# A fused attention and two-MLP kernel: stacked hi/lo heads in the feature projection, folds moved from VectorE to GpSimd, weight work reordered

## The chip, the cores and the metric

The kernel runs on one core of a Trainium2 chip. The metric is the device time of one execution in microseconds (us), from which the median of several executions is quoted.

## What is computed

Three layers follow each other, for 4 batches of 576 tokens with 512 features.

```python
proj = einsum('bhsd,df->bhsf', x, w_phi)            # 8 heads of 64, 128 features
proj = proj - max(abs(proj), axis=-1)
phi  = concatenate([exp(proj), exp(-proj)])         # for q and for k
kv, z = phi(k)^T v, sum(phi(k))
attn = phi(q) kv / (phi(q) z + 1e-6)
x  = attn as (4, 576, 512)
u  = x + real(fft(fft(x, axis=1), axis=2))
x  = u + relu(layernorm(u) @ w_ch1) @ w_ch2         # 512 -> 2048 -> 512
u  = x + (relu(x^T @ w_tok1) @ w_tok2)^T            # over tokens, 576 -> 256 -> 576
out = u + relu(u @ w_ch1') @ w_ch2'                 # 512 -> 1536 -> 512
```

Nearly every product is made of three passes in the type fp32r: a number is split into a rounded part `hi` and a rest `lo`, and hi·hi, hi·lo and lo·hi are summed in PSUM.

## The kernel before, in words

**Attention** (`front`). Two heads of a batch make a pair; there are 16 pairs, four for a batch, and a step for each. All engines run the same list of steps, each in its own order, tied by semaphores. Step k on TensorE (`pe_step`, L421) projects the five token groups of pair k+1 (units REST, KA, KB, QA, QB; REST has one tile of 128 tokens, the others two, so nine tiles in a pair) and, between them, turns the query features of pair k (`pe_turn`), forms `kv` (`pe_kv`) and forms `num` (`pe_num`). The last two are in plain f32, for which one matmul of the program shows as two records in the trace. Between the units stand pieces of the Fourier transform of the batch before (`pe_piece`, in the steps where k % 4 is 1, 2 or 3).

In `pe_project` (L286) the 128 rows of a tile hold the features of both heads, and `wphi` is block diagonal, so 256 columns come out, 128 for each head. Three matmuls of 256 columns are made for a tile: hi with `wphi_hi`, hi with `wphi_lo`, lo with `wphi_hi`. `qk_hi` is rounded on ScalarE three steps ahead (`act_round`), `qk_lo` is the rest, made on GpSimd (`pool_split`). Each unit goes to one of two PSUM banks, so it waits (`shifted`) until VectorE has read the unit before the last one.

VectorE subtracts the largest absolute value (`dve_shift`), divides (`dve_norm`) and, for the transform, forms sums of mirrored tokens (`dve_sum`) and of mirrored features (`dve_even`); GpSimd forms the differences (`pool_fold`) and adds the finished transform to x (`pool_add`, `pool_row`). SyncE's queue issues the loads (`load_qk`, `load_v`) and the stores of u (`store`), in the order in which they are written, each behind its waits.

**First MLP** (`channel_mlp`, NF1 = 16 chunks j of hidden features; 6 blocks of 384 tokens). `early_vector` makes the mean and variance of block 0 (`early_stats`) and its reciprocal root and normed values (`early_norm`, which calls `dve_first_rstd`) while attention still runs. During block 0 the last batch's transform is still under way, and the weights come in: SyncE loads a chunk to one of four buffers, ScalarE rounds it (`act_weights`), GpSimd makes the rest (`mlp1["gpsimd"](pool, waits, first, stop)`). The sequence on GpSimd after the last step is written out in `gpsimd`:

```python
mlp1["gpsimd"](pool, (), 4, 6)
pool_add(pool, LAST, 0)
pool_add(pool, LAST, 1)
mlp1["gpsimd"](pool, ((7, u_stored[2], 32),), 6, 8)
pool_add(pool, LAST, 2)
pool_row(pool, LAST)
mlp1["gpsimd"](pool, ((13, u_stored[3], 32),), 8)
```

**Token MLP** (`token_mlp`). Its second weight `w2` is loaded by SyncE once all of the first MLP's outputs are made (`y_done`), into memory that the first MLP's weights held, then rounded on ScalarE and split on VectorE; TensorE's second product waits for it.

## Time and profile before

| | us |
|---|---|
| median of 3 runs (lowest, highest) | 994.19 (993.21, 994.72) |
| the profiled execution, its own time | 993.24 |
| its span in the trace, first to last instruction | 991.4 |
| TensorE busy in it (matmul records) | 976.3 |
| VectorE, ScalarE, GpSimd busy | 380.3, 285.3, 181.6 |
| mean granted TensorE clock, as a share of full speed | 0.998 |

The profiled execution lies 1.84 us above its span and 0.95 us under the median. A matmul's record is longer than the time to the next matmul, since they overlap, so a busy share of 98% does not say how many stalls there are; the starts of successive records, and the bracket at a record's end that names the idle time before it and what ended it, say that. Attention takes the time up to about 200 us, the first MLP up to about 624, the token MLP up to about 680, and the second MLP the rest.

### The profile page before, as it was taken

The numbers are of one execution on the slowest core, as the hardware profiler recorded it, in microseconds if no ns is written. First come the engines' busy times: TensorE is split into PE (matmuls) and PEld (weight loads), VectorE is DVE, ScalarE is ACT, GpSimd is POOL, SyncE is SP. The second block draws the span as 40 slices with busy tenths as digits, with TensorE's granted clock in tenths as the row PEclk, the third lists the DMA queues.
The fourth block names the chain that finished last, engine by engine and source line by source line (L and its number), as shares of the span: only waits on it lengthen the run. The fifth ranks groups of instructions, "written<-read, shape, count | busy, mean of one in ns | idle before, by whom it ended". The sixth has DMA issues, their size and how long they took to land.

```text
span 991.4 us, 17316 instructions
## 1 busy us (share of the span) xinstructions
PE 976.3 (98%) x7275; PEld 879.4 (89%) x7275; DVE 380.3 (38%) x758; ACT 285.3 (29%) x573; POOL 181.6 (18%) x159
## 2 busy tenths in 40 slices
PE   8999999999999999999999999999999999999998
PEld 6999999888899999899899999788999999999997
DVE  6998888851421322313213213463121212121211
ACT  6865756633311111111111112353111111111110
POOL 3653555369500000000000000136000000000000
PEclk9999999999999999999999999999999999999999
DMA  7232241435310010010100300695010101000000
GB/s 230 80 111 55 74 130 48 165 110 166 108 64 1 1 64 1 1 63 0 37 26 0 105 7 1 208 322 197 1 64 1 64 1 51 13 33 30 32 1 32
DMA packets 48398, 66.88 MB, mean 67 GB/s; under 512 B 22864, under 2 KB 23888, under 8 KB 48208
## 3 DMA queue, kind: packets, MB, share of 16 engines
q1 hardware_dynamic: 46608, 59.69, 18.6%
q10 hardware_dynamic: 1728, 6.29, 1.7%
q8 instruction: 48, 0.79, 0.3%
q14 instruction: 14, 0.11, 0.0%
HBM read 47.10 MB, written 18.87 MB: 67 GB/s over the span
## 4 chain that ended last, share of the span: by engine, by line
PE 73%; POOL 2%; DMA 1%; DVE 1%; ACT 0%; issue 0%; SPq 0%; POOLq 0%
PE mlp_y L1086 11%; PE mlp_y L1087 11%; PE mlp_hid L1073 11%; PE mlp_hid L1071 11%; PE mlp_hid L1072 11%; PE mlp_y L1085 11%; PE mlp_turn_in L1056 1%; PE tok_y L1387 1%; PE tok_y L1389 1%; PE tok_y L1388 1%; POOL mlp_w_lo L1033 1%; DMA mlp_w_raw<-in_w_mlp 1%; PE tok_hid L1389 1%; PE tok_hid L1388 1%; PE tok_hid L1387 1%; DMA tok_w<-in_w_tok 0%
## 5 line engine op out<-in xcount | busy, mean ns | idle before, releaser
L1204 DVE SCALAR_TENSOR_TENSOR mlp_h_lo<-mlp_hid,mlp_h_hi 128x384 fp32r<-128x384 f32 x168 | 93.7, 558 | 465.1 <-ACT mlp_h_hi L1121 465.0
L1071 PE MATMUL mlp_hid<-mlp_ut_hi,mlp_w_hi 128*128 128x384 f32 x672 | 229.1, 341 | 0.5 <-POOL mlp_w_lo L1033 0.5
L1121 ACT ACTIVATE mlp_h_hi<-mlp_hid 128x384 fp32r<-128x384 f32 x168 | 82.7, 492 | 502.9 <-PE mlp_hid L1073 502.9
L1073 PE MATMUL mlp_hid<-mlp_ut_hi,mlp_w_lo 128*128 128x384 f32 x672 | 226.5, 337 | 0.0
L1072 PE MATMUL mlp_hid<-mlp_ut_lo,mlp_w_hi 128*128 128x384 f32 x672 | 225.4, 335 | 0.0
L1085 PE MATMUL mlp_y<-mlp_w_hi,mlp_h_hi 128*128 128x512 f32 x504 | 197.3, 391 | 3.0 <-DVE mlp_h_lo L1204 2.9
L1087 PE MATMUL mlp_y<-mlp_w_hi,mlp_h_lo 128*128 128x512 f32 x504 | 199.4, 396 | 0.0
L1086 PE MATMUL mlp_y<-mlp_w_lo,mlp_h_hi 128*128 128x512 f32 x504 | 198.9, 395 | 0.0
L1033 POOL TENSOR_TENSOR mlp_w_lo<-mlp_w_raw,mlp_w_hi 128x1024 fp32r<-128x1024 f32 x26 | 61.7, 2395 | 402.9 <-ACT mlp_w_hi L1282 381.6
L1071 PEld LDWEIGHTS mlp_hid<-mlp_ut_hi,mlp_w_hi 128*128 128x128 f32 x672 | 126.3, 188 | 6.6 <-issue 1.2
L1072 PEld LDWEIGHTS mlp_hid<-mlp_ut_lo,mlp_w_hi 128*128 128x128 f32 x672 | 126.3, 188 | 5.2
L1073 PEld LDWEIGHTS mlp_hid<-mlp_ut_hi,mlp_w_lo 128*128 128x128 f32 x672 | 126.0, 188 | 0.0
L1087 PEld LDWEIGHTS mlp_y<-mlp_w_hi,mlp_h_lo 128*128 128x128 f32 x504 | 94.5, 187 | 20.4
L1085 PEld LDWEIGHTS mlp_y<-mlp_w_hi,mlp_h_hi 128*128 128x128 f32 x504 | 94.7, 188 | 19.0 <-issue 2.1
L1086 PEld LDWEIGHTS mlp_y<-mlp_w_lo,mlp_h_hi 128*128 128x128 f32 x504 | 94.6, 188 | 15.9
L629 DVE TENSOR_REDUCE absmax<-proj 128x4 f32<-128x512 f32 (+1 forms) x80 | 50.7, 634 | 15.4 <-PE proj L299 14.6
L1190 DVE TENSOR_TENSOR mlp_ut_lo<-mlp_turn_in,mlp_ut_hi 128x384 fp32r<-128x384 f32 x44 | 24.5, 558 | 75.0 <-ACT mlp_ut_hi L1114 74.9
L637 DVE TENSOR_TENSOR pm<-proj,absmax 128x512 f32<-128x512 f32 (+1 forms) x80 | 51.1, 638 | 4.7
L297 PE MATMUL proj<-wphi_hi,qk_hi 128*128 128x256 f32 x144 | 46.7, 324 | 3.8 <-DVE wphi_lo L758 1.8
L494 ACT ACTIVATE eq<-pt 128x512 f32<-128x512 f32 (+1 forms) x96 | 42.0, 491 | 26.1 <-PE pt L312 25.9
L480 ACT ACTIVATE ek<-pm 128x512 f32<-128x512 f32 (+1 forms) x96 | 48.4, 559 | 1.5 <-DVE pm L637 1.5
L786 POOL TENSOR_TENSOR qk_lo<-qk,qk_hi 128x576 fp32r<-128x576 f32 x30 | 42.1, 1423 | 16.7 <-ACT qk_hi L467 16.7
(146 smaller groups left out, 1081.9 us busy)
## 6 DMA issues: line engine op xcount, KB each, us to landing
mlp_u<-u_scratch SPq DMA_DIRECT2D x12, 768.0 KB, 4.6
mlp_w_raw<-in_w_mlp SPq DMA_DIRECT2D x14, 512.0 KB, 5.2
mlp_w_raw<-in_w_mlp ACTq DMA_DIRECT2D x12, 512.0 KB, 6.0
v<-in_v SPq DMA_DIRECT2D x16, 320.0 KB, 3.6
qk<-in_kT SPq DMA_DIRECT2D x16, 288.0 KB, 4.1
qk<-in_qT SPq DMA_DIRECT2D x15, 288.0 KB, 4.2
...
```

The costliest lines, as they stand in the source:

```text
L480: last = nc.scalar.activation(out, in_, ACT.Exp, scale=(1.0, -1.0)[sign])
L629: nc.vector.tensor_reduce(absmax[:, unit, 0:cols], src, AX.X, ALU.max, apply_absolute_value=True).then_inc(absmax_done, 1)
L637: nc.vector.tensor_tensor(pm[p.parity][:, unit, 0:cols, :], src, top, ALU.subtract).then_inc(shifted, 1)
L1033: nc.gpsimd.tensor_tensor(w_lo[:, nf - 1 - j, :], raw(j), w_hi[:, j, :], ALU.subtract).then_inc(w_split, 1)
L1071: nc.tensor.matmul(out, w_hi[:, j, col], hi, start=(c == 0), stop=False)
L1072: nc.tensor.matmul(out, w_hi[:, j, col], lo, start=False, stop=False)
L1073: last = nc.tensor.matmul(out, w_lo[:, nf - 1 - j, col], hi, start=False, stop=(c == DC - 1))
L1085: nc.tensor.matmul(y[t][:, :], hi, w_hi[:, j, D:2 * D], start=(j == 0), stop=False)
L1086: nc.tensor.matmul(y[t][:, :], hi, w_lo[:, nf - 1 - j, D:2 * D], start=False, stop=False)
L1087: last = nc.tensor.matmul(y[t][:, :], lo, w_hi[:, j, D:2 * D], start=False, stop=(j == nf - 1))
L1121: nc.scalar.activation(h_hi[:, j % 2, :], hid[j % 2][:, 0:BT], ACT.Relu).then_inc(h_rounded, 1)
L1204: nc.vector.scalar_tensor_tensor(out=h_lo[:, j % 2, :], in0=hid[j % 2][:, 0:BT], scalar=0.0, in1=h_hi[:, j % 2, :], op0=ALU.max, op1=ALU.s ...
```

## The change

Five edits. (1) From pair 1 on a tile is projected by `qk_lo` with `wphi_hi` (256 columns) and then, for each head, by one matmul of 128 columns: the 128 rows of its weights hold the head's 64 rounded features twice (`rest_twice`, `key_twice`, `query_twice`), and `wphi_both` holds the rounded `w_phi` above its rest. The doubled features are copies from SBUF to SBUF, twelve DMAs for a pair on SyncE's queue, and REST, KA and QA wait for them. Keys and queries have one buffer each, REST has two. The transform table is loaded behind the copies of pair 1. (2) Sums of mirrored tokens and features go from VectorE to GpSimd, but for the last pair's, which the two engines share; `pool_add` calls come a step later or behind the fold, and the stores of batch 0 and 1 later. (3) Statistics and root of the first MLP block go to the units s = 2 and s = 3 of step 14. (4) Five weight loads stand ahead of the last store, not three, and GpSimd makes rests 6 to 9 ahead of adds. (5) `w2` and its parts lie elsewhere in memory, are loaded four chunks before the end of the first MLP and split during its last chunks.

```diff
+    wphi_both = at("wphi_both", [128, F], F32R, 157824)
+    rest_twice = at("rest_twice", [128, 2, 2, 128], F32R, 134912)
+    key_twice = at("key_twice", [128, 2, 512], F32R, 130816)
+    query_twice = at("query_twice", [128, 2, 512], F32R, 77824)
...
+    def copy_twice(sp, p, first, to, done):
+        for h in range(2):
+            for half in range(2):
+                from_ = qk_hi[DH * h:DH * h + DH, p.parity, first:first + to.shape[2]]
+                sp.dma_start(to[64 * half:64 * half + 64, h, :].bitcast(F32), from_.bitcast(F32)).then_inc(done, 16)
+
+    def copy_rest(sp, p):
+        wait_if(sp, proj_done, 5 * p.n - 9 if p.n >= 3 else 0)
+        sp.wait_ge(qk_rounded, 2 * p.n + 2)
+        copy_twice(sp, p, FIRST[REST], rest_twice[:, p.parity], rest_copied[p.parity])
+
+    def copy_keys(sp, p):
+        wait_if(sp, proj_done, 5 * p.n - 2 if p.n >= 2 else 0)
+        copy_twice(sp, p, FIRST[KA], key_twice, key_copied)
+
+    def copy_queries(sp, p):
+        wait_if(sp, proj_done, 5 * p.n if p.n >= 2 else 0)
+        copy_twice(sp, p, FIRST[QA], query_twice, query_copied)
...
+        sp.wait_ge(qk_rounded, 3)
+        copy_keys(sp, Pair(1))
+        copy_rest(sp, Pair(1))
+        copy_queries(sp, Pair(1))
...
+            copy_rest(sp, Pair(n))
+            copy_keys(sp, Pair(n))
             load_v(sp, Pair(n))
-            if n in (11, 15):
-                store(sp, n // 4 - 2)
+            copy_queries(sp, Pair(n))
+            if n == 13:
+                store(sp, 0)
...
         mlp1["load_block"](sp, 0)
+        store(sp, 1)
         sp.wait_ge(u_stored[1], 32)
...
-        mlp1["load_weights"](sp, 8, [0, 1, 2])
+        mlp1["load_weights"](sp, 8)
+        mlp1["load_weights"](sp, 12, [0, 1])
         store(sp, 3)
-        mlp1["load_weights"](sp, 8, [3])
-        mlp1["load_weights"](sp, 12)
+        mlp1["load_weights"](sp, 12, [2, 3])
...
+        if p.n > 0 and unit == REST:
+            pe.wait_ge(rest_copied[p.parity], 64 * ((p.n + 1) // 2))
+        if p.n > 0 and unit == KA:
+            pe.wait_ge(key_copied, 64 * p.n)
+        if p.n > 0 and unit == QA:
+            pe.wait_ge(query_copied, 64 * p.n)
...
-            nc.tensor.matmul(out, hi, wphi_hi[:, :], start=True, stop=False)
-            nc.tensor.matmul(out, hi, wphi_lo[:, :], start=False, stop=False)
-            last = nc.tensor.matmul(out, lo, wphi_hi[:, :], start=False, stop=True)
+            if p.n == 0:
+                nc.tensor.matmul(out, hi, wphi_hi[:, :], start=True, stop=False)
+                nc.tensor.matmul(out, hi, wphi_lo[:, :], start=False, stop=False)
+                last = nc.tensor.matmul(out, lo, wphi_hi[:, :], start=False, stop=True)
+                continue
+            first = 256 * (unit in (KB, QB)) + 128 * j
+            nc.tensor.matmul(out, lo, wphi_hi[:, :], start=True, stop=False)
+            for h in range(2):
+                last = nc.tensor.matmul(out[:, F * h:F * h + F], twice[:, h, first:first + 128], wphi_both[:, :],
+                                        start=False, stop=(h == 1))
...
+                pe.wait_ge(wphi_rounded, 2)
+                pe.wait_ge(wphi_split, 2)
...
+        nc.scalar.copy(wphi_both[0:DH, :], wphi[0:DH, 0:F]).then_inc(wphi_rounded, 1)
...
-    def dve_sum(dve, p):
...
-        x = x_of(b)
+    def dve_last_fold(dve):
+
+        cols = slice(D - 2 * DH, D)
+        dve.wait_ge(x_done, PAIRS)
+        dve.wait_ge(odd_folded, 2 * B - 1)
+        x = x_of(LAST)
         nc.vector.tensor_tensor(fold_s[:, :, cols], x[:, 0:FRONT, cols], x[:, 5:2:-1, cols],
                                 ALU.add).then_inc(summed, 1)
-
-    def dve_even(dve, b, i):
-        dve.wait_ge(summed, 4 * b + 3 + i)
-        low, high = MIRROR[i]
+        low, high = MIRROR[1]
+        dve.wait_ge(summed, PAIRS)
         nc.vector.tensor_tensor(fold_s[:, :, low], fold_s[:, :, low], fold_s[:, :, high],
                                 ALU.add).then_inc(even_folded, 1)
...
-                for n in ready(k):
-                    if k < PAIRS - 1:
-                        dve_fold(dve, Pair(n))
-            if s == 4 and k == PAIRS - 2:
+            if s == 2 and k == PAIRS - 2:
                 mlp1["early_vector"][0](dve)
+            if s == 3 and k == PAIRS - 2:
+                mlp1["early_vector"][1](dve)
             if s == 0 and k == PAIRS - 1:
                 dve.wait_ge(proj_done, 5 * PAIRS)
-                mlp1["early_vector"][1](dve)
-            if s == 4 and k == PAIRS - 1:
-                dve_fold(dve, Pair(k - 1))
+                mlp1["early_vector"][2](dve)
...
+        nc.vector.tensor_tensor(wphi_both[DH:128, :], wphi[DH:128, F:2 * F], wphi_hi[DH:128, F:2 * F],
+                                ALU.subtract).then_inc(wphi_split, 1)
...
-        pool.wait_ge(summed, p.n + 1)
-        if i >= 2:
-            pool.wait_ge(even_folded, 2 * b + i - 1)
+        pool.wait_ge(x_done, p.n + 1)
         if b > 0:
             pool.wait_ge(fold_split, 2 * b)
         x = x_of(b)
+        nc.gpsimd.tensor_tensor(fold_s[:, :, cols], x[:, 0:FRONT, cols], x[:, 5:2:-1, cols],
+                                ALU.add).then_inc(summed, 1)
         nc.gpsimd.tensor_tensor(fold_d[:, :, cols], x[:, 0:FRONT, cols], x[:, 5:2:-1, cols],
                                 ALU.subtract).then_inc(differed, 1)
         if i >= 2:
+            low, high = MIRROR[i - 2]
+            pool.wait_ge(summed, p.n + 1)
+            nc.gpsimd.tensor_tensor(fold_s[:, :, low], fold_s[:, :, low], fold_s[:, :, high],
+                                    ALU.add).then_inc(even_folded, 1)
             pool.wait_ge(differed, p.n + 1)
-            low, high = MIRROR[i - 2]
+            pool.wait_ge(even_folded, 2 * b + i - 1)
...
+        cols = slice(D - 2 * DH, D)
+        pool.wait_ge(x_done, PAIRS)
+        pool.wait_ge(odd_folded, 2 * B - 1)
+        x = x_of(LAST)
+        nc.gpsimd.tensor_tensor(fold_d[:, :, cols], x[:, 0:FRONT, cols], x[:, 5:2:-1, cols],
+                                ALU.subtract).then_inc(differed, 1)
...
+        pool.wait_ge(edge_made, 2 * B)
+        nc.gpsimd.tensor_tensor(fold_d[:, :, low], fold_d[:, :, low], fold_d[:, :, high],
+                                ALU.subtract).then_inc(odd_folded, 1)
...
+        if k % 4 == 2 and b >= 1:
+            pool_add(pool, b - 1, 2)
+            pool_row(pool, b - 1)
+        if k > 0:
+            pool_fold(pool, Pair(k - 1))
         if k % 4 == 3 and 0 <= b < LAST - 1:
             pool_add(pool, b, 0)
-        if k % 4 == 0 and b >= 1:
+        if k % 4 == 1 and b >= 1:
             pool_add(pool, b - 1, 1)
-        for n in ready(k):
-            pool_fold(pool, Pair(n))
-        if k % 4 == 1 and b >= 1:
-            pool_add(pool, b - 1, 2)
-            pool_row(pool, b - 1)
...
+        pool_last_fold(pool)
...
+        mlp1["gpsimd"](pool, ((7, u_stored[2], 32),), 6, 8)
         pool_add(pool, LAST, 1)
-        mlp1["gpsimd"](pool, ((7, u_stored[2], 32),), 6, 8)
+        mlp1["gpsimd"](pool, (), 8, 10)
         pool_add(pool, LAST, 2)
         pool_row(pool, LAST)
-        mlp1["gpsimd"](pool, ((13, u_stored[3], 32),), 8)
+        mlp1["gpsimd"](pool, ((13, u_stored[3], 32),), 10)
...
-        dve_first_rstd(dve)
...
+    def sync_middle(sp):
+        sp.dma_start(w2[:, :, :], dram["w_tok2"].rearrange("(c p) s -> p c s", p=128)).then_inc(w2_loaded, 16)
+
     def sync_low(sp):
-        sp.dma_start(w2[:, :, :], dram["w_tok2"].rearrange("(c p) s -> p c s", p=128)).then_inc(w2_loaded, 16)
...
+        if step == 5:
+            act.wait_ge(w2_loaded, 16)
+            nc.scalar.copy(w2_hi[:, :, :], w2[:, :, :]).then_inc(w_rounded, 1)
...
-        act.wait_ge(w2_loaded, 16)
-        nc.scalar.copy(w2_hi[:, :, :], w2[:, :, :]).then_inc(w_rounded, 1)
...
+        if step == 4:
+            dve.wait_ge(w_rounded, 2)
+            nc.vector.tensor_tensor(w2_lo[:, :, :], w2[:, :, :], w2_hi[:, :, :], ALU.subtract).then_inc(w_split, 1)
...
-        dve.wait_ge(w_rounded, 2)
-        nc.vector.tensor_tensor(w2_lo[:, :, :], w2[:, :, :], w2_hi[:, :, :], ALU.subtract).then_inc(w_split, 1)
...
-            sp.wait_ge(*mlp1["y_done"])
+            sp.wait_ge(*mlp1["hid_to"](NF1 - 4))
+            tok["sync_middle"](sp)
+            sp.wait_ge(*mlp1["hid_to"](NF1))
             tok["sync_low"](sp)
```

The projection on TensorE, in step 4, from the REST unit of pair 5 to the first matmul of its KA unit, before:

```order
L297 MATMUL proj<-wphi_hi,qk_hi 128x256 [waits shifted,qk_split,table_split]
L298 MATMUL proj<-wphi_lo,qk_hi 128x256
L299 MATMUL proj<-wphi_hi,qk_lo 128x256
L312 MATMUL pt<-mlp_ident,pm_102 128x128 [waits shifted,qexp_done]
L312 MATMUL pt<-mlp_ident,pm_102 128x128 x3
L297 MATMUL proj<-wphi_hi,qk_hi 128x256 [waits shifted]
```

and the same units of pair 3 in the changed kernel:

```order
L342 MATMUL proj<-wphi_hi,qk_lo 128x256 [waits shifted,rest_copied1,qk_split]
L344 MATMUL proj<-wphi_both,rest_twice 128x128 x2
L358 MATMUL pt<-mlp_ident,pm_106 128x128 [waits shifted,qexp_done]
L358 MATMUL pt<-mlp_ident,pm_106 128x128 x3
L342 MATMUL proj<-wphi_hi,qk_lo 128x256 [waits shifted,key_copied]
```

A tile is still three matmuls, two of them half as wide, and the units wait for the copies too. What SyncE issues between the loads of one pair and the next, before:

```order
L230 DMA qk<-in_kT 128x576 [waits qk_split]
L231 DMA qk<-in_qT 128x576
L238 DMA v<-in_v 128x10x64 [waits kv_done]
L230 DMA qk<-in_kT 128x576 [waits qk_split]
L231 DMA qk<-in_qT 128x576
```

and in the changed kernel:

```order
L235 DMA qk<-in_kT 128x576 [waits qk_split]
L236 DMA qk<-in_qT 128x576
L249 DMA rest_twice<-qk_hi 64x128 [waits qk_rounded,proj_done]
L249 DMA rest_twice<-qk_hi 64x128 x3
L249 DMA key_twice<-qk_hi 64x512 [waits proj_done]
L249 DMA key_twice<-qk_hi 64x512 x3
L243 DMA v<-in_v 128x10x64 [waits kv_done]
L249 DMA query_twice<-qk_hi 64x512 [waits proj_done]
L249 DMA query_twice<-qk_hi 64x512 x3
```

Fifteen DMAs now stand where three stood. GpSimd in the last steps, from the fold of pair 14 to the first weight rest behind it, before:

```order
L798 TENSOR_TENSOR fold<-x_all 128x3x128 [waits fold_split,even_folded,summed]
L806 TENSOR_TENSOR fold<-fold 1x127 [waits differed]
L808 TENSOR_TENSOR fold<-fold 128x3x127 [waits edge_made]
L868 COPY fold<-fold 1x2 [waits even_folded,last_differed,odd_folded]
L869 TENSOR_TENSOR fold<-fold 1x128
L1033 TENSOR_TENSOR mlp_w_lo<-mlp_w_raw,mlp_w_hi 128x1024 [waits mlp1_w_rounded,fold_split]
```

and in the changed kernel:

```order
L820 TENSOR_TENSOR fold<-x_all 128x3x128 [waits fold_split,x_done]
L822 TENSOR_TENSOR fold<-x_all 128x3x128
L827 TENSOR_TENSOR fold<-fold 128x3x127 [waits summed]
L834 TENSOR_TENSOR fold<-fold 1x127 [waits even_folded,differed]
L836 TENSOR_TENSOR fold<-fold 128x3x127 [waits edge_made]
L845 TENSOR_TENSOR fold<-x_all 128x3x128 [waits odd_folded,x_done]
L851 COPY fold<-fold 1x2 [waits even_folded,differed]
L852 TENSOR_TENSOR fold<-fold 1x128
L854 TENSOR_TENSOR fold<-fold 128x3x128 [waits edge_made]
```

Four more operations stand on GpSimd there, and VectorE keeps two of the last pair's.

## Rows read from the trace of the kernel before

**Rows 1.** Stretches: us, busy of PE, PEld, DVE, ACT, POOL; PEclk, DMA share, GB/s.
```profile
8.00:10.00 2.00, 2.00 (x11) 1.95 (x9) 1.58 (x4) 1.28 (x3) 1.45 (x2) 0.50 1.20 219
...
24.00:185.00 161.00, 159.45 (x2793) 149.47 (x2793) 141.00 (x291) 106.69 (x239) 85.10 (x88) 1.00 0.32 95
```
**Rows 2.** Timeline of PE, two projection matmuls inside a unit: start us, us, engine, line.
```profile
63.46 0.28 PE L298 MATMUL proj<-wphi_lo,qk_hi 128*128 128x256 f32 x1
63.58 0.28 PE L299 MATMUL proj<-wphi_hi,qk_lo 128*128 128x256 f32 x1
```
**Rows 3.** Timeline of PEld, the first two weight loads of that unit.
```profile
63.24 0.19 PEld L297 LDWEIGHTS proj<-wphi_hi,qk_hi 128*128 128x128 f32 x1 [0.39 <-DVE pm L637]
63.35 0.19 PEld L298 LDWEIGHTS proj<-wphi_lo,qk_hi 128*128 128x128 f32 x1
```
**Rows 4.** Chain that ended last, three turns of 128 columns: start us, us, what.
```profile
268.40 0.33 PE mlp_turn_in L1056 x3
```
**Rows 5.** Waits of PE: us in total, times, longest; whole span, then 24 to 195.
```profile
PE proj L297 <- DVE wphi_lo L758: 1.8, 1, 1.8
...
PE proj L297 <- DVE pm L637: 0.6, 3, 0.2
```
**Rows 6.** Groups of DVE and of POOL, 24 to 195 us: busy, mean ns, idle before.
```profile
L668 DVE TENSOR_TENSOR fold<-x_all 128x384 f32<-128x384 f32 x14 | 8.2, 584 | 0.5
L674 DVE TENSOR_TENSOR fold<-fold 128x381 f32<-128x381 f32 (+1 forms) x6 | 3.3, 557 | 0.2
```
```profile
L798 POOL TENSOR_TENSOR fold<-x_all 128x384 f32<-128x384 f32 x14 | 14.1, 1007 | 55.7 <-DVE fold L668 49.9 <-DVE fold L674 5.7
```
**Rows 7.** Timelines of PE, ACT and SyncE's queue (SPq) near the start.
```profile
13.20 0.36 PE L297 MATMUL proj<-wphi_hi,qk_hi 128*128 128x256 f32 x1 [0.44 <-DVE pm L637]
```
```profile
9.24 0.65 ACT L467 CAST qk_hi<-qk 128x576 fp32r<-128x576 f32 x1
```
```profile
8.64 0.43 SPq L231 DMA_DIRECT2D qk<-in_qT  x1
9.12 0.43 SPq L258 DMA_DIRECT2D table<-in_table  x1
```
**Rows 8.** The tensor qk: time from a DMA's issue to its landing.
```profile
DMA to landing us min/median/max: 2.5/4.2/7.9
```
**Rows 9.** Timeline of PE, steps 1 and 2: two `num`, and QA between.
```profile
30.39 2.09 PE L340 MATMUL num<-kvs,eq 128*64 128x65 f32 x64
...
38.34 0.36 PE L297 MATMUL proj<-wphi_hi,qk_hi 128*128 128x256 f32 x1
...
39.94 2.09 PE L340 MATMUL num<-kvs,eq 128*64 128x65 f32 x64
```
**Rows 10.** Timelines of PE and DVE in step 15, around the first MLP's root.
```profile
196.11 0.52 PE L1056 MATMUL mlp_turn_in<-mlp_ident,mlp_un 128*128 128x128 f32 x3 [1.21 <-DVE mlp_ut_lo L1190]
```
```profile
188.96 0.16 DVE L1167 TENSOR_SCALAR mlp_rstd<-mlp_var_eps 128x3 int32<-128x3 int32 x1
...
191.13 1.46 DVE L1185 TENSOR_SCALAR mlp_un<-mlp_u,mlp_mean_var,mlp_rstd 128x512 f32<-128x512 f32 x3
```
**Rows 11.** Timelines of PE and DVE after the last pair.
```profile
206.28 0.47 PE L1085 MATMUL mlp_y<-mlp_w_hi,mlp_h_hi 128*128 128x512 f32 x1 [1.85 <-DVE mlp_h_lo L1204]
```
```profile
204.98 0.56 DVE L695 TENSOR_TENSOR fold<-fold 128x384 f32<-128x384 f32 x1 [0.84 <-POOL fold L869]
```
**Rows 12.** Chain that ended last and timeline of PE, at the last store of u.
```profile
244.51 6.89 DMA mlp_w_raw<-in_w_mlp
```
```profile
245.95 0.41 PE L1071 MATMUL mlp_hid<-mlp_ut_hi,mlp_w_hi 128*128 128x384 f32 x1 [0.46 <-POOL mlp_w_lo L1033]
...
253.50 0.50 PE L1085 MATMUL mlp_y<-mlp_w_hi,mlp_h_hi 128*128 128x512 f32 x1 [1.02 <-DVE mlp_h_lo L1204]
```
**Rows 13.** Chain that ended last, and waits of PE, at the token MLP.
```profile
624.43 3.99 DMA tok_w<-in_w_tok
```
```profile
PE tok_y L1387 <- DVE tok_h_lo L1450: 1.0, 1, 1.0
```

More of the change, by code:

```diff
@@ L153, in front @@
     qk_split = sem("qk_split")
+    rest_copied = [sem("rest_copied0"), sem("rest_copied1")]
+    key_copied = sem("key_copied")
+    query_copied = sem("query_copied")
     proj_done = sem("proj_done")
@@ L290, in pe_project @@
             pe.wait_ge(qk_split, 2 * p.n + 2)
+        if p.n > 0 and unit == REST:
[4 more added lines that the diff above has]
+            pe.wait_ge(query_copied, 64 * p.n)
         wait_if(pe, shifted, 5 * p.n + unit - 1)
         out_bank = proj[(p.parity + unit) % 2]
+        twice = {REST: rest_twice[:, p.parity], KA: key_twice, KB: key_twice, QA: query_twice, QB: query_twice}[unit]
         for j in range(1 if unit == REST else 2):
```

54 lines of the change are left out of this document (17 added, 37 removed).

## The prediction

> **What bounds the kernel now.** I read the stretches first: between 24 and 185 us TensorE has a record open for 159.45 of 161.00 us, VectorE works 141.00, ScalarE 106.69, GpSimd 85.10, and the DMA engines are busy 0.32 of the time [rows 1]. So TensorE carries attention, VectorE is near behind, GpSimd has room. The list of TensorE's waits says how little it waits there: 0.6 us in all for VectorE's shift [rows 5]. An edit can therefore pay in two ways only: by making TensorE's own stream shorter, or by filling one of the few holes, of which the larger ones lie at the change to the first MLP, at the last store and at the token MLP [rows 10 to 13]. What the stream costs is read from the starts of successive records, not from their lengths. A matmul of 256 columns inside a unit takes 0.12 us to the next [rows 2]. The first two weight loads of a unit, which nothing hinders, lie 0.11 us apart [rows 3], and three turns of 128 columns take 0.33 us, 0.11 each [rows 4]. Hence a load of 128 columns of weights takes 0.11 us, and 256 columns of data just cover it.
>
> **1, projection.** For pairs 1 to 15 there are 135 tiles, each with one matmul of 256 columns as before and two of 128 in place of 256: 270 narrow ones. The data of a narrow one would pass in half of 0.12, 0.06 us, but each still has a weight load of its own, of 128 columns, and nothing is left to cover it. I take 0.11 us for it, since both rows with 128 columns of weights show that. It saves 270 x 0.01 = 2.7 us. The ends: if the data alone set the pace, 270 x 0.06 = 16 us saved; if fp32r this narrow costs more than its columns, a loss, since no row shows fp32r under 256 columns; the size is worked out with the rivals.
> The Trainium skill (TensorE: Matmul & The Clock Gate, Back-to-back issue gap) puts a sustained stream of weight loads and 128-column matmuls at about 81 ns each. By that figure, as an estimate, the saving would be 270 x 39 ns = 10.5 us; the rows here show 110 ns for such pairs, and I go by them.
>
> **1, copies in mid-run.** SyncE's queue issues a DMA in 0.48 us (8.64 to 9.12) [rows 7]. Twelve more make 5.8 us, fifteen 7.2 us for a pair, under the shortest step, 9.55 us (30.39 to 39.94) [rows 9]. The tightest chain is that of the queries, with one buffer: it is free when QB of the pair before is projected, just ahead of num at 30.39, and the next QA starts at 38.34 [rows 9], 8 us later. Four issues are 1.9 us, and a landing takes 4.2 us in the middle [rows 8]: 6.1 us, so about 2 us are left. The keys have a like chain. In bytes a pair's copies are 1.18 MB, 110 GB/s over a mean step of 161/15 = 10.7 us; the rows give 0.32 share for 95 GB/s [rows 1], so the share goes to about 0.7. I take nothing for mid-run. The cover is the 2 us; with the longest landing, 7.9 us [rows 8], it is gone and each short step pays 1.7 us.
>
> **1, the start.** Here the copies are not ahead. TensorE projects REST of pair 1 at 13.20 us; its features are rounded at 9.9 (9.24 + 0.65), and the queue is free at 9.12, where it issued the table [rows 7]. Now the four key copies go first (to 11.0), then the four of REST (to 13.0), and with a landing of 2.5 to 4.2 us [rows 8] REST starts at 15.5 to 17.2. TensorE runs in order, so this is a hole of 2.2 to 4 us. REST's copies are small and I take the short landing; 0.2 us of later waits for VectorE vanish in it: 2.0 us lost. The table lands later by some 6 us, but ScalarE comes to it only at the end of step 0; the loads behind it have more than a step. Pair 0's extra cast and subtraction lie where both engines wait for loads: nothing, and 0.3 us without that cover.
>
> **2, folds.** VectorE loses 8.2 + 3.3 us of work, GpSimd gains twenty operations of 1.0 us and had 55.7 us of idle ahead of these folds, ended by the very sums that it now makes itself [rows 6]. It goes from 85 to about 105 us of 161. What TensorE can get back is its wait for the shift, 0.6 us as the list counts it, and the short starts of units that it doesn't count; I take 1.0, ends 0 and 2.
>
> **3, root.** The chain of small operations from 188.96 to 191.13 us on VectorE, 2.2 us, leaves step 15. Behind it stood the split for which TensorE waited 1.21 us [rows 10]. The statistics now delay the shift of QA and QB in step 14 by some 3 us, but these feed turns that come a step part later. I take 1.2; ends 0 and 1.4. Late next would be that split again, behind the division.
>
> **2, last fold.** TensorE waits 1.85 us for the first h_lo, which stands on VectorE behind a fold that waits for GpSimd (204.98, idle 0.84) [rows 11]. That fold goes to GpSimd, one difference too, and VectorE keeps two operations of 0.56. The split can then follow the ScalarE cast at once: 1.6 of the 1.85. GpSimd has four more operations ahead, but its fold of pair 14 can start earlier with the root, so the rounded folds come no later.
>
> **4, weight loads.** One load takes 6.89 us behind the store of 1 MB, ScalarE waits for it with a cast in hand, and TensorE loses 1.02 us for it; 0.46 us more go by a rest that GpSimd made behind its adds [rows 12]. Both are moved ahead: 1.5 us, ends 0.5 and 1.8. The store lands later, and chunk 13 waits for it, two chunks from then.
>
> **5, token MLP.** The load of w2, 3.99 us, starts only at 624.43, and TensorE waits 1.0 us at the end of that chain [rows 13]. Loaded four chunks earlier it is out of the way, and the casts fit between chunks of over 4 us: 1.0 us.
>
> **The sum.** -2.7 + 2.0 - 1.0 - 1.2 - 1.6 - 1.5 - 1.0 = -7.0 us. The profiled execution took 993.24 us for a span of 991.4, and lies 0.95 us under the median of the runs; its 993.2 becomes 986.2, the median 994.2 becomes 987.2.
>
> **The rivals.**
> *Narrow fp32r is dear* (slower). Plain f32 shows that type sets the number of passes: 32 matmuls of num in the program are 64 records [rows 9]. If a matmul of 128 columns in fp32r took two loads' time, 0.22 us, a tile would cost 0.12 + 0.44 for 0.36: 135 x 0.20 = 27 us more, and 2.7 not gained: 1017 us. It decides from 0.136 us for a narrow matmul, where 4.3 us of other gains are used up. For it: no row excludes it. Against it: the turns, also 4-byte data, keep to 0.11. Chance 0.12.
> *Copies late in every short step.* With landings of 7.9 us, five short steps give 8.5 us: 996; in every pair, 15 x 1.7 = 25 us: 1013. It decides when copies land over 6.2 us after their last issue. Against it: the DMA engines stay under full. Chance 0.12, of which 0.05 stay within the bound.
> *The hole at the start costs the clock.* The clock was granted at 0.50, the 1.2 GHz level, between 8 and 10 us [rows 1], after TensorE had waited 1.8 us [rows 5]. If the new hole does it again, some 4 us pass at half speed, 2 us more: 989.2. Chance 0.08.
> *The waits come back elsewhere*: GpSimd, or VectorE in step 14, is late, and edits 2 to 4 give a third of their 5.3 us: 990.7. Chance 0.05.
> *Weight loads overlap more than the rows show*: narrow matmuls take 0.06 and 16.2 us are saved instead of 2.7: 973.7. Chance 0.05. By the 81 ns of the Trainium skill's page, as an estimate, it would be 979.
>
> **How the numbers follow.** The forecast itself has 0.58, with 984 to 991 as its own range (start 1 to 5, holes 2 to 7, projection 1 to 4). To hold 8 in 10 the range takes in the clock, the returning waits and the milder late copies: 982 to 997. About 0.2%, 2 us, is what a measurement of this kernel can tell from no change. Faster by more: 0.58 + 0.08 + 0.05 and 0.03 of the returning waits, 0.74. Within: 0.05 of the late copies, 0.02 of the returning waits, 0.07. Slower: 0.12 + 0.07 = 0.19.
>
> **What would show it.** Starts of narrow matmuls 0.11 us apart and steps of 9.4 us instead of 9.55; REST of pair 1 starting at 15 to 16 us, with the copies as releaser, and no wait for copies after step 1; VectorE's busy time 12 us lower, GpSimd's 25 higher; TensorE's waits for h_lo under 0.7 us in all, none at the turns of block 0, none before tok_y. Wrong would be: 0.06 or over 0.13 us between narrow matmuls; waits of QA or KA for copies in step after step; ScalarE idle before the table's cast.

## The result and the profile after

| | before | changed |
|---|---|---|
| median (lowest, highest), 19 runs each, us | 994.02 (992.6, 995.2) | 998.57 (994.73, 1000.96) |
| ratio to before, 95% interval | | 1.0047 [1.0038, 1.0055] |
| profiled execution, us; its span | 993.24; 991.4 | 998.46; 996.6 |
| GpSimd, VectorE busy, us | 181.6, 380.3 | 204.8, 373.5 |

The changed kernel is slower by 0.5%, 4.6 us, where 7 us less were forecast; the time lies above the range. The runs of the changed kernel lie 6.2 us apart, those of before 2.6; nothing here settles what spreads them, and each view below is of one execution. The first view I read is the stretches of the changed kernel (columns as in [rows 1]).

```profile
12.00:14.00 2.00, 1.23 (x7) 1.01 (x6) 1.91 (x3) 1.88 (x4) 0.00 (x0) 0.86 0.80 206
14.00:16.00 2.00, 0.00 (x0) 0.01 (x1) 0.76 (x2) 0.51 (x1) 1.92 (x2) 1.00 0.31 77
16.00:18.00 2.00, 1.97 (x10) 2.00 (x11) 0.85 (x2) 0.19 (x1) 0.84 (x1) 0.50 0.88 203
18.00:20.00 2.00, 2.00 (x11) 2.00 (x11) 0.98 (x2) 1.50 (x4) 0.00 (x0) 0.50 1.04 261
20.00:22.00 2.00, 2.00 (x24) 1.67 (x25) 1.69 (x3) 0.86 (x2) 0.00 (x0) 0.50 1.03 429
...
24.00:185.00 161.00, 153.15 (x2761) 144.12 (x2758) 125.60 (x258) 105.62 (x234) 100.03 (x103) 0.99 0.74 186
...
44.00:54.00 10.00, 8.00 (x153) 7.46 (x153) 6.85 (x15) 6.68 (x15) 6.96 (x7) 1.00 0.76 178
...
74.00:76.00 2.00, 2.00 (x23) 1.67 (x23) 1.86 (x4) 0.81 (x2) 0.17 (x1) 0.50 0.95 283
```

TensorE stands for the whole of 14 to 16 us, and then works at a granted clock of 0.50, the 1.2 GHz level, up to some 22.5 us. At 74 us the clock is down once more. In attention it is busy 153 of 161 us where it was 159 [rows 1]. The list of its waits over the whole span says for what:

```profile
PE proj L342 <- DMA key_twice<-qk_hi: 6.4, 5, 2.5
PE proj L342 <- DMA rest_twice<-qk_hi: 2.8, 1, 2.8
PE mlp_y L1126 <- DVE mlp_h_lo L1245: 1.3, 2, 0.8
```

The 2.8 us are the hole at the start, ahead of REST of pair 1. The 6.4 us are five waits of KA. That hole and the two longest of the five, from TensorE's timeline:

```profile
16.03 0.55 PE L342 MATMUL proj<-wphi_hi,qk_lo 128*128 128x256 f32 x1 [2.79 <-DMA rest_twice<-qk_hi]
...
50.74 0.38 PE L342 MATMUL proj<-wphi_hi,qk_lo 128*128 128x256 f32 x1 [2.00 <-DMA key_twice<-qk_hi]
...
72.64 0.38 PE L342 MATMUL proj<-wphi_hi,qk_lo 128*128 128x256 f32 x1 [2.46 <-DMA key_twice<-qk_hi]
```

Why the keys are late is read from SyncE's queue, here in steps 1 and 2, one pair's fifteen DMAs and the first of the next:

```profile
29.72 3.25 SPq L249 DMA_DIRECT2D rest_twice<-qk_hi  x4
33.01 2.52 SPq L249 DMA_DIRECT2D key_twice<-qk_hi  x4
35.58 0.61 SPq L243 DMA_DIRECT2D v<-in_v  x1
36.23 4.17 SPq L249 DMA_DIRECT2D query_twice<-qk_hi  x4
40.44 0.58 SPq L235 DMA_DIRECT2D qk<-in_kT  x1
41.06 0.44 SPq L236 DMA_DIRECT2D qk<-in_qT  x1
41.61 2.82 SPq L249 DMA_DIRECT2D rest_twice<-qk_hi  x4
```

The queue goes from one DMA straight to the next, yet from one pair's first copy to the next pair's 11.9 us pass (29.72 to 41.61). Four copies take at least 2.5 us, 0.64 each from one to the next, and the other three groups shown take 0.3 to 1.7 us more. A short step of TensorE (k = 1 to 4, 8 and 12) lasts 9.3 to 9.55 us when nothing holds it, so the queue falls behind in steps 1 to 4, which follow each other.

I then took from each profile the start of the last record of num in every step, in us. Their distances are the lengths of the steps, long ones where pieces of the transform stand in them; "edits 2 to 5" and "half the DMAs" are experiments told below.

```
                 step 0 ends   lengths of steps 1 to 15                                                     step 15 ends
before              22.94   9.55  9.55  9.55 10.29 11.30 15.07 13.48 9.55 11.29 15.04 13.48 9.55 11.29 15.04 12.85   199.83
changed             28.10   9.47 10.00 11.39 10.04 14.66 14.88 13.31 9.30 11.09 14.86 13.31 9.31 11.76 14.86 12.72   209.06
edits 2 to 5        23.35   9.55  9.55  9.55  9.55 11.00 15.04 13.48 9.55 10.98 15.07 13.49 9.55 11.00 15.07 12.65   198.44
half the DMAs       27.61  11.55  9.31  9.31  9.31 11.10 14.86 13.31 9.31 11.08 14.88 13.31 9.31 11.09 14.86 12.72   202.91
```

Against before, the changed kernel loses 5.16 us up to the end of step 0 and 4.07 in steps 1 to 15, and gains 4.03 behind them (span less the last column: 791.57, then 787.54). The sum, 5.20, is the difference of the spans.

### The profile page after: what moved, and what is told of

Its sections match the earlier page's. It is cut to its first block, busy times and chain, and to the rows that moved or that the text cites. A ratio compares the mean times of both kernels' runs of the same rounds, so it can differ in the third digit from the quotient of the medians.

```text
span 996.6 us, 17539 instructions
## 1 busy us (share of the span) xinstructions
PE 977.5 (98%) x7275; PEld 881.0 (88%) x7275; DVE 373.5 (37%) x735; ACT 285.6 (29%) x574; POOL 204.8 (21%) x183
## 4 chain that ended last, share of the span: by engine, by line
PE 75%; DVE 1%; ACT 0%; issue 0%; DVEq 0%
PE mlp_y L1127 11%; PE mlp_hid L1114 11%; PE mlp_y L1128 11%; PE mlp_hid L1112 11%; PE mlp_hid L1113 11%; PE mlp_y L1126 11%; PE mlp_turn_in L1097 1%; PE tok_y L1433 1%; PE tok_y L1434 1%; PE tok_y L1435 1%; PE tok_hid L1433 1%; PE tok_hid L1434 1%; PE tok_hid L1435 1%; DVE mlp_var_eps L1183 1%; DVE mlp_u L1237 0%; PE tok_hid L1454 0%
## 5 line engine op out<-in xcount | busy, mean ns | idle before, releaser
L342 PE MATMUL proj<-wphi_hi,qk_lo 128*128 128x256 f32 x135 | 47.3, 351 | 9.3 <-DMA key_twice<-qk_hi 6.4
L810 POOL TENSOR_TENSOR qk_lo<-qk,qk_hi 128x576 fp32r<-128x576 f32 x30 | 42.0, 1418 | 15.5 <-ACT qk_hi L515 9.8
```

## Experiments

My theory was that edit 1 holds the whole loss, in two places: the hole at the start with the clock behind it, and a queue that issues too slowly. The rivals: the moved folds cost something; the single key buffer, or bytes, or the DMA engines make the copies late; the narrow matmuls are dear. Each run was timed beside the kernel before on its chip, and ratios are against that.

**Edits 2 to 5 alone.** The projection and the queue of before, everything else changed.

```diff
+    NEW = []
...
     def copy_keys(sp, p):
+        if p.n not in NEW:
+            return
...
-            if p.n == 0:
+            if p.n not in NEW:
                 nc.tensor.matmul(out, hi, wphi_hi[:, :], start=True, stop=False)
```

> The changed kernel with the projection of before and no copies, so edits 2 to 5 alone. Theory (the whole loss is edit 1's: a hole at the start with the clock halved behind it, and key copies that come late): attention ends near 199 us, and the holes that edits 3 to 5 fill give about 4 to 5 us, so 989 to 990 us. Rival (moving the folds and the statistics costs something in attention, so that the loss is not all edit 1's): 993 or more, with new waits for VectorE or GpSimd in the steps.

Measured: 987.30 us against 993.77, ratio 0.9934 [0.9921, 0.9946]. All the loss is edit 1's, 11 us of it beside these edits, and 987.3 is some 2 us under what I expected: steps 4, 5, 9 and 13 are shorter by 1.64 us in all (the table). Of edits 2 to 5 only edit 2, the moved folds, is at work in these steps.

**Edit 1 alone**, put into the kernel before: copies, waits, narrow matmuls, the table behind the copies.

> The kernel before with edit 1 alone (doubled copies, two matmuls of 128 columns in place of 256-column hi products). Theory: it takes the start's 5 us and the late key copies' 4 us and gives nothing else back: 1002 to 1004 us. Rival (copies and moved folds disturb each other, for instance at the SBUF or through GpSimd's rests): clearly under 1001, since VectorE and GpSimd have the old division of work.

Measured: 1001.55 us, ratio 1.0082 [1.0066, 1.0098], 7.8 us slower, just under what the theory said. Waits for key copies 4.8 us, for REST 2.9 us, with the old division of work between VectorE and GpSimd. So the late copies don't come from the moved folds. That is 3 us less than edit 1 costs beside the others, of which 1.6 are the shorter waits for keys; the rest stays open.

**Pair 1 projected as before**, copies from pair 2 on.

```diff
+    NEW = range(2, PAIRS)
```

> The changed kernel, but pair 1 is projected as before and needs no copies; the queue is then about 8 us further on when it comes to pair 2. Theory (the start's 5.2 us are the hole and the half clock behind it; the later waits for key copies come from a queue that issues 15 DMAs in 10.8 us where a short step lasts 9.3): the first num ends near 23 us, and a head start of 8 us of queue time covers the lag of 1.5 us a step through steps 1 to 4, so the waits for key copies shrink from 6.4 us to under 2: 987 to 990 us. Rival (the single key buffer, not the queue's rate, makes the copies late): the start is mended, the waits of steps 2 to 5 stay: 993 us.

Measured: 992.14 us, ratio 0.9990 [0.9979, 1.0001]. Step 0 ends at 23.22, so the start is mended, 4.9 us. The key waits fall from 6.4 to 3.5 us and don't go under 2: the head start is soon used up, and one wait of 1.7 us stands in step 13, behind the store of batch 0 in the same queue. The time lies between the theory's (987 to 990) and the rival's (993): the head start was worth less than I took it for.

**Half the DMAs**, from pair 3 on.

```diff
-            for half in range(2):
+            for half in range(2 if p.n < 3 else 1):
```

> The changed kernel, but from pair 3 on only the first half of each doubled operand is copied: two DMAs in place of four for each of rest, keys and queries. It leaves out the second halves, so the hi with w_lo products of pairs 3 to 15 use stale features. Nine DMAs a pair in place of fifteen. Theory (queue's issue rate): 9 issues take about 6.5 us, the queue catches up within two steps; the waits for key copies from step 3 on vanish, and with them the half clock at 74 to 77 us; the start's loss stays: 991 to 993 us. Rival (the single buffer or the latency of a copy): waits stay, 997 or more.

Measured: 992.07 us, ratio 0.9984 [0.9973, 0.9996]. The list of waits of TensorE, up to 215 us, has for the keys

```profile
PE proj L342 <- DMA key_twice<-qk_hi: 0.3, 1, 0.3
```

and no step from 2 to 15 is lengthened (table), with the same single buffers. That rules out the single buffers as what makes the copies late. Beside the row of edits 2 to 5 it also gives the saving of the narrow matmuls: 0.24 us in short steps, 0.17 to 0.21 in long ones, and a loss of 0.1 in steps 5, 9 and 13, where num now waits 0.5 us for VectorE's x_all.

**Count against bytes.** The run above halved both. Two more part them: one with as many DMAs of half the columns, one with the same bytes in half the DMAs (128 partitions, straight across).

```diff
+        cols = to.shape[2] if p.n < 3 else to.shape[2] // 2
-                from_ = qk_hi[DH * h:DH * h + DH, p.parity, first:first + to.shape[2]]
+                from_ = qk_hi[DH * h:DH * h + DH, p.parity, first:first + cols]
-                sp.dma_start(to[64 * half:64 * half + 64, h, :].bitcast(F32), from_.bitcast(F32)).then_inc(done, 16)
+                sp.dma_start(to[64 * half:64 * half + 64, h, 0:cols].bitcast(F32), from_.bitcast(F32)).then_inc(done, 16)
```

> The changed kernel, but from pair 3 on each copy takes only the first half of its columns: as many DMAs as before (15 a pair with the loads), half the bytes in the copies. It leaves out the second halves (KB, QB and half of REST of pairs 3 to 15 use stale doubled features). Theory (the count of issues, 0.64 us each, is the limit): the queue still needs over 10 us a pair, the waits for key copies stay over 4 us, 996 to 999 us. Rival (bytes or landing time is the limit): they vanish as in the run with half the DMAs, 991 to 993 us.

```diff
+        if p.n >= 3:
+            for h in range(2):
+                from_ = qk_hi[:, p.parity, first:first + to.shape[2]]
+                sp.dma_start(to[:, h, :].bitcast(F32), from_.bitcast(F32)).then_inc(done, 16)
+            return
```

> The changed kernel, but from pair 3 on each doubled operand is filled by two DMAs over 128 partitions in place of four over 64: the same bytes, nine DMAs a pair in place of fifteen. It leaves out the doubling, since both halves come straight across (rows 64 to 127 hold the other head). Together with the runs of half the DMAs and of half the columns this parts count from bytes. Theory (the count of DMAs on the queue is the limit): a wide one is issued in 0.6 us too, a pair's issues take under 9 us, the waits for key copies vanish: 991 to 993 us. Rival (bytes and rows of the copies): four issues' worth of time stays, waits over 4 us: 996 to 999 us.

Measured: half the columns 996.06 us, ratio 1.0028 [1.0019, 1.0037], key waits 3.1 us; half the count 991.45 us, ratio 0.9978 [0.9969, 0.9988], key waits 0.4 us. SyncE's queue, half the columns first, then half the count:

```profile
42.22 3.36 SPq L250 DMA_DIRECT2D rest_twice<-qk_hi  x4
45.63 2.95 SPq L250 DMA_DIRECT2D key_twice<-qk_hi  x4
...
53.59 2.39 SPq L250 DMA_DIRECT2D rest_twice<-qk_hi  x4
```

```profile
39.17 1.11 SPq L249 DMA_DIRECT2D rest_twice<-qk_hi  x2
40.47 1.13 SPq L249 DMA_DIRECT2D key_twice<-qk_hi  x2
43.43 0.58 SPq L243 DMA_DIRECT2D v<-in_v  x1
45.10 1.12 SPq L249 DMA_DIRECT2D query_twice<-qk_hi  x2
```

With half the bytes a pair still takes the queue 11.4 us (42.22 to 53.59). With all the bytes in half the DMAs (each over 128 partitions) each is issued in the same 0.56 us, and the queue has pauses. The count is what binds. The run before these and the first of these move the same bytes over the same 64 partitions and differ in the count alone: 0.3 us of key waits there, 3.1 here. It is not quite all: with half the bytes the waits halved too, which the theory had not expected (waits over 4 us). Between 28 and 70 us key copies landed in 2.3 us instead of 2.4, too little for it; where the rest comes from stays open.

**Queries issued by ScalarE's queue**, from pair 2 on.

```diff
-            copy_queries(sp, Pair(n))
...
             if s == 0:
                 if k >= 0:
                     act_qexp(act, p, 0)
+                if 2 <= following < PAIRS:
+                    act.wait_ge(qk_rounded, 2 * following + 2)
+                    copy_queries(act, Pair(following), nc.scalar)
```

> The changed kernel, but from pair 2 on the four query copies of a pair are issued by ScalarE's queue at the start of the step in which they are used. SyncE's queue then has 11 DMAs a pair, about 7.5 us. Theory (rate of one queue is the limit): waits for key copies vanish, the start stays lost, ScalarE loses about 2.5 us a step of which it has 3 to 4 idle: 991 to 994 us. Rival (the DMA engines or the single buffers are the limit): waits for key or query copies stay, 997 or more. Second rival: ScalarE becomes late with its exponentials, TensorE waits for pm or for the query copies in each short step, over 999 us.

Measured: 1011.49 us, ratio 1.0177 [1.0162, 1.0192]. The theory holds as far as the keys go, their waits are down to 0.4 us. The second rival wins. ScalarE's queue and TensorE's waits:

```profile
56.02 0.47 ACTq L250 DMA_DIRECT2D query_twice<-qk_hi  x1
56.51 1.91 ACTq L250 DMA_DIRECT2D query_twice<-qk_hi  x3
58.53 0.72 ACT L528 ACTIVATE ek<-pm 64x256 f32<-64x256 f32 x2 [1.49 <-DVE pm L689]
```

```profile
PE proj L342 <- DMA query_twice<-qk_hi: 5.8, 5, 2.2
PE pt L354 <- ACT eq L542: 5.4, 5, 1.8
```

The exponentials stand behind four issues of 0.6 us, and the query copies behind the exponentials. These two waits are 11.2 us, and the mean granted clock from 24 to 185 us is 0.96 where it was 0.99. The Trainium skill (DMA: Bandwidth & Descriptors, Issuing engines are not separate DMA queues) says that issuing from several engines saves only the sequencer's time to start a DMA, "usually small relative to the DMA itself". Here it is not small: four issues (2.5 us) are about as long as a landing (2.6 us in the middle), and in the changed kernel the sum of a pair's issues is the limit.

**REST copied first** for pair 1.

> The changed kernel with the order of pair 1's copies turned: REST, then keys. Theory (a hole of 2.2 us cost no clock at 48 us, holes of 2.6 and 3.0 us did): REST starts near 14.3 us after a hole of 1.3 us, KA near 17.3 after one of 1.9; no hole reaches 2.6 us, the clock stays at 1.0, and the first num ends near 26 us, so 996.5 us. Rival (the clock falls after the idle time of both together): half clock from 17 us on, first num at 28 us as before, 998.5 us.

Measured: 999.59 us, ratio 1.0050 [1.0037, 1.0064]. My theory of the clock fell. Two holes came as forecast, neither over 2 us, and the clock fell all the same:

```profile
14.32 0.36 PE L342 MATMUL proj<-wphi_hi,qk_lo 128*128 128x256 f32 x1 [1.18 <-DMA rest_twice<-qk_hi]
...
17.14 0.41 PE L342 MATMUL proj<-wphi_hi,qk_lo 128*128 128x256 f32 x1 [1.83 <-DMA key_twice<-qk_hi]
```

```profile
16.00:18.00 2.00, 0.86 (x5) 0.87 (x6) 0.00 (x0) 1.03 (x3) 0.75 (x1) 0.84 0.90 205
18.00:20.00 2.00, 2.00 (x11) 2.00 (x11) 1.42 (x3) 0.00 (x0) 0.00 (x0) 0.50 1.04 228
```

The length of a hole didn't tell whether the clock would fall behind it. With pair 1 projected as before it fell behind a hole of 1.05 us, with one of 0.39 two us ahead of it; in this run, later on, it stayed through one of 2.78 (the first pair of lines below is from the former, the second from the latter):

```profile
54.88 0.39 PE L352 MATMUL proj<-wphi_hi,qk_lo 128*128 128x256 f32 x1 [1.05 <-DMA key_twice<-qk_hi]
56.00:58.00 2.00, 2.00 (x11) 1.78 (x10) 1.83 (x3) 0.00 (x0) 2.00 (x2) 0.50 1.02 252
...
52.95 0.39 PE L342 MATMUL proj<-wphi_hi,qk_lo 128*128 128x256 f32 x1 [2.78 <-DMA key_twice<-qk_hi]
54.00:56.00 2.00, 2.00 (x46) 1.83 (x46) 1.88 (x3) 0.95 (x2) 2.00 (x3) 1.00 0.97 265
```

So a hole can be charged with a price for the clock only where a trace shows the fall.

**The hole filled.** Twelve dummy matmuls ahead of REST of pair 1.

```diff
+                for n in range(12):
+                    nc.tensor.matmul(num[:, 512 * (n % 2):512 * (n % 2) + 512], warm[:, 0:128], warm[:, :],
+                                     start=True, stop=True)
```

> The changed kernel with 12 warm-up matmuls (512 columns, bf16, into the bank of num, which nothing uses yet) ahead of pair 1's REST, where TensorE waited 3.0 us for the copies: they add no time if they end before the copies land. Theory (of the 5 us lost at the start 3 are the hole and some 2.4 the half clock behind it, since step 0 took 12.1 us from REST to the last num and 9.7 before): the clock stays at 1.0 after 16 us, the first num ends near 25.6 us; the queue is not faster, so up to 2 us of it come back as waits for key copies in steps 1 to 4: 996 to 998.5 us. Rival (the clock falls whatever TensorE does there, for instance because of the DMA traffic): 0.50 from 16 to 22 us as before, first num at 28 us, 998.5 us.

Measured: 997.92 us, ratio 1.0042 [1.0029, 1.0055].

```profile
12.45 2.76 PE L503 MATMUL num<-warm 128*128 128x512 bf16 x12
15.77 0.36 PE L342 MATMUL proj<-wphi_hi,qk_lo 128*128 128x256 f32 x1 [0.55 <-issue]
...
28.16 0.36 PE L342 MATMUL proj<-wphi_hi,qk_lo 128*128 128x256 f32 x1 [2.81 <-issue]
```

```profile
16.00:18.00 2.00, 2.00 (x19) 1.97 (x19) 1.43 (x3) 1.21 (x3) 0.23 (x1) 1.00 0.90 208
18.00:20.00 2.00, 2.00 (x54) 1.83 (x55) 1.93 (x4) 1.81 (x5) 0.00 (x0) 1.00 0.97 258
```

The clock stays at 1.00 and step 0 ends at 25.13 us instead of 28.10. So TensorE's idleness made the clock fall, not the DMA traffic, and that cost 2.7 us: from REST to the last num step 0 took 12.07 us, here 9.36. The Trainium skill (TensorE: Matmul & The Clock Gate, HAM oscillation — how this bites in real kernels) describes this, a wait for a DMA after which the next stretch runs at half the clock, and these two traces agree. But the gain was gone at once: step 1 took 14.15 us, since REST of pair 2 has to wait until 28.16, and behind that hole the clock fell after all (granted 0.51 from 30 to 32 us). Its copies were issued up to 21.4 us, behind 1.5 MB of table, and from 16 to 30 us DMAs landed late (issues, KB each, median us to landing):

```profile
table<-in_table SPq DMA_DIRECT2D x1, 1512.0 KB, 7.5
...
rest_twice<-qk_hi SPq DMA_DIRECT2D x5, 32.0 KB, 5.9
```

In the changed kernel this second lateness was hidden behind the first (REST of pair 2 at 28.25). That the table causes it is argued from these rows; no run moved the table alone.

**Copies for the later pairs only**: from pair 6, and from pair 4, with the store of batch 0 a step later.

```diff
+    NEW = range(6, PAIRS)
...
-            if n == 13:
+            if n == 14:
                 store(sp, 0)
```

> Edits 2 to 5, and edit 1 for pairs 6 to 15 alone; the store of batch 0 one step later. The short steps at the start keep the old projection, so there is no hole at 13 us and no backlog. Theory (a pair with copies that come in time saves 0.17 to 0.24 us, as the steps of the run with half the DMAs show): 987.3 - 10 x 0.2 = 985.3 us. Rival (the queue is late in steps 12 and 13 too, 1.9 us there in the run with pair 1 projected the old way): 986.5 to 988 us.

> Edits 2 to 5, and edit 1 for pairs 4 to 15 (before: 6 to 15 gave 986.6 us). Pairs 4 and 5 are projected in two more short steps. Theory (the queue falls some 1.5 us behind in each short step and has 2 us of slack): two short steps in a row are just covered, each saves 0.24 us more: 986.1 us, waits for copies under 0.5 us in all. Rival (no slack: the copies are late from the first short step on): a wait of 1 to 2 us for key copies in step 4 or 5, 987 to 988 us.

Measured: from pair 6 986.61 us, ratio 0.9926 [0.9913, 0.9939], no wait for copies in the list; from pair 4 988.31 us, ratio 0.9946 [0.9932, 0.9960], key waits 2.2 us, of which

```profile
63.77 0.39 PE L352 MATMUL proj<-wphi_hi,qk_lo 128*128 128x256 f32 x1 [1.76 <-DMA key_twice<-qk_hi]
```

stands in step 5, behind two short steps with copies; the rival without slack was right. With long steps between, the copies come in time. The last num of attention starts at 197.17 with edit 1 from pair 6 and at 198.44 without it; as a time the gain, 0.7 us, is not told apart by the intervals. In this profile a wait of 0.6 us stands ahead of tok_y, which edit 5 had removed; with edits 2 to 5 alone and in the changed kernel it is not there.

**Edit 3 undone**, beside edits 2, 4 and 5.

> Edits 2, 4 and 5 alone: the run with the old projection, with edit 3 undone too (statistics at the end of step 14, root and normed values in step 15). Theory (edit 3 only moves a wait: the hole of 1.4 us before the turns of block 0 became one of 0.3 us there and one of 0.9 us at the transform's piece before it, behind VectorE): within 0.4 us of the run with edit 3, 987.2 to 987.8 us, the last num of attention 0.2 us later. Rival (edit 3 is worth its 1.2 us, and the 0.9 us hole is there without it): 988.5 us.

Measured: 987.86 us, ratio 0.9940 [0.9927, 0.9953], 0.2 us later at the last step (12.84 against 12.65). TensorE's waits around the root, undone first, then as changed:

```profile
194.07 0.52 PE L1101 MATMUL mlp_turn_in<-mlp_ident,mlp_un 128*128 128x128 f32 x3 [1.21 <-DVE mlp_ut_lo L1235]
```

```profile
199.49 0.38 PE L397 MATMUL four<-table_hi,ab_hi 128*128 128x258 f32 x1 [0.71 <-DVE more L745]
```

Without edit 3 the second wait is not there; with it, in the run of edits 2 to 5 as well, the second is there (0.7 us) and the first has no bracket any more. The root's 2.2 us only moved ahead of QB's shift and of the sums of the transform (`more`), whose bank TensorE then wants.

**A held operation on VectorE.** In the changed kernel, and in the runs with all of edit 4, TensorE waits 0.8 us for h_lo at 268 us. VectorE's timeline there, and GpSimd's:

```profile
261.09 6.46 DVE L1183 TENSOR_SCALAR mlp_var_eps<-mlp_mean_var 128x2 f32<-128x2 f32 x1
...
267.73 0.55 DVE L1245 SCALAR_TENSOR_TENSOR mlp_h_lo<-mlp_hid,mlp_h_hi 128x384 fp32r<-128x384 f32 x1
```

```profile
255.69 11.82 POOL L1074 TENSOR_TENSOR mlp_w_lo<-mlp_w_raw,mlp_w_hi 128x1024 fp32r<-128x1024 f32 x5
```

Two numbers a partition take 6.46 us (1.74 before), and end with GpSimd's row of five rests (255.69 + 11.82 = 267.51). One run puts the order of the rests back, in the version of edits 2 to 5 alone; the other makes the addition column by column, in the version from pair 6.

```diff
         pool_add(pool, LAST, 0)
+        pool_add(pool, LAST, 1)
         mlp1["gpsimd"](pool, ((7, u_stored[2], 32),), 6, 8)
-        pool_add(pool, LAST, 1)
-        mlp1["gpsimd"](pool, (), 8, 10)
         pool_add(pool, LAST, 2)
         pool_row(pool, LAST)
-        mlp1["gpsimd"](pool, ((13, u_stored[3], 32),), 10)
+        mlp1["gpsimd"](pool, ((13, u_stored[3], 32),), 8)
```

> Edits 2 to 5 without edit 1, and of edit 4 only the order of the weight loads: GpSimd makes rests 6 to 9 in the order of the kernel before. Theory (five rests in a row on GpSimd hold VectorE's 128x2 addition for 6.5 us, and TensorE waits 0.8 us for the h_lo behind it): rests and adds alternate again, the addition takes under 3 us, the 0.8 us wait goes, and a wait of 0.4 to 0.5 us for a rest comes back: within 0.5 us of the run with edit 4 whole (987.3 us). Rival (the addition is held by something else, a semaphore or the statistics of another place): it stays at 6.5 us, the 0.8 us wait stays and 0.5 us are added: 987.8 us.

```diff
-            nc.vector.tensor_scalar(var_eps[:, 0:t], mean_var[:, 0:t, 1], 1e-6, None, ALU.add)
+            for c in range(t):
+                nc.vector.tensor_scalar(var_eps[:, c:c + 1], mean_var[:, c:c + 1, 1], 1e-6, None, ALU.add)
```

> The version with edit 1 for pairs 6 to 15 (986.6 us), with the addition of epsilon to the variances made as 128x1 operations, one for each column, in place of one of 128x2. Theory (the held instruction is held for its form, which wants what GpSimd holds; one column is not of that form): each takes some 0.15 us, h_lo is not late, the 0.8 us wait goes: 985.8 us. Rival (any operation of VectorE that reads and writes SBUF alone is held while GpSimd works): the first column takes over 6 us, 986.6 us, or a little more for the extra instruction.

Measured: rests as before 987.37 us, ratio 0.9929 [0.9916, 0.9943]; by column **985.60 us, ratio 0.9915 [0.9901, 0.9928]**, the lowest median of all, 8.4 us under before. It lies 1.0 us under the version from pair 6, but the two intervals overlap; what shows the effect is the trace. Its VectorE and GpSimd:

```profile
249.26 0.21 DVE L1194 TENSOR_SCALAR mlp_var_eps<-mlp_mean_var 128x1 f32<-128x1 f32 x2
```

```profile
243.85 11.83 POOL L1084 TENSOR_TENSOR mlp_w_lo<-mlp_w_raw,mlp_w_hi 128x1024 fp32r<-128x1024 f32 x5
```

In the same place, beside the same row of rests, two columns take 0.21 us and the 0.8 us wait is gone. Behind attention this trace takes 786.5 us, where the changed kernel took 787.5. With the rests as before the addition of 128x2 took 0.86 us, the wait for h_lo went and 0.5 us for a rest came back, as the theory had it. The Trainium skill (SBUF — State Buffer, SBUF: two separate sides) says that VectorE in some of its modes and GpSimd take a port in turn, each for a whole instruction. The traces agree that one waits for the other. They show more: the addition began at 261.09, within the third of the five rests (2.36 us each), and VectorE did not get its turn between GpSimd's instructions, it waited to the end of the fifth.

## Why the prediction was wrong

**Copies in mid-run, taken at nothing: the step that failed.** "SyncE's queue issues a DMA in 0.48 us" came from loads near the start [rows 7] and was carried over to copies; these take 0.64, and groups of four are held up to 1.7 us more. The trace of before had it already, further on: a pair's three loads take the queue 1.8 us (19.16 to 20.97), 0.6 each.

```profile
19.16 0.55 SPq L238 DMA_DIRECT2D v<-in_v  x1
19.75 0.75 SPq L230 DMA_DIRECT2D qk<-in_kT  x1
20.54 0.43 SPq L231 DMA_DIRECT2D qk<-in_qT  x1
```

A pair's fifteen DMAs therefore take 10.1 to 11.9 us instead of 7.2, more than a short step. And the chain that I worked out was that of the queries; "the keys have a like chain" was not worked out, and the keys were the late ones, since REST's copies and the loads stand ahead of them. The cover of 2 us was worked out with a queue that is free when it is wanted, and it was not. From start to start TensorE's five holes ahead of KA sum to 7.2 us (6.4 in the list of waits), and step 5, with the longest, is 3.7 us over its 11.0, some 1 us more than its hole; the clock, at 0.50 from 74 to 76 us, goes with it. The rival of late copies (996 to 1013 us) takes in the measured time, but by slow landings, over 6.2 us; they landed in 2.5. Its mechanism was wrong, and that its range fits is luck. I had the count and the step length side by side: fifteen DMAs at 0.6 us are 9 us, against a step of 9.55, and leave nothing for a group that is held.

**The start, 2.0 us lost: 5.2.** REST started at 16.03, inside the 15.5 to 17.2 forecast, a hole of 2.8. The rival "the hole costs the clock" came true beside it, at 2.3 us net where 2 were written: from REST to the last num step 0 took 12.07 us, before 9.74, and 9.36 with the hole filled. That rival had 0.08. The trace had already shown such a fall, after a wait of 1.8 us [rows 1, 5], so it deserved more.

**Projection, 2.7 us saved: about 2.0.** The price was right. A tile takes 0.34 us in place of 0.36 (groups of the timeline at 29.73 and 30.07 us), three weight loads of 0.11, so a narrow fp32r matmul costs its weight load. Its sign was not: the starts within a tile lie 0.17, 0.06 and 0.11 us apart, and by "0.06 between narrow matmuls", taken alone, the tile would have looked cheaper than it is. Both rivals on the price (0.22; 0.06) are out by the length of the tile. So are the 81 ns of the Trainium skill (TensorE: Matmul & The Clock Gate, Back-to-back issue gap): the trace has 0.11 us for such a pair. But three steps gave nothing, being VectorE's by then.

**Folds 1.0: 1.6**, within the ends; GpSimd's busy time rose by 23 us, VectorE's fell by 6.8, which is 11.5 less the 4.7 that the held addition took more (6.46 against 1.74).

**Root 1.2: 0.2.** "Late next would be that split again" named the wrong one: late next was the transform's `more`.

**Last fold 1.6: 1.4** (wait for h_lo 1.85 [rows 11], now 0.49). **Weight loads 1.5:** both waits [rows 12] are gone, and 0.8 came back through the held addition. **Token MLP 1.0:** the wait [rows 13] is gone.

Together edits 2 to 5 were forecast at 6.3 us and gave 6.5. The forecast was wrong by edit 1 alone: 0.7 gained by its terms, some 11 us lost.
